# Windowed attention and a gated feed-forward layer on one core: pooled scores in one product, shorter turns, another order of the outputs

## The reference

```python
# q, k, v: (4 batches, 8 heads, 576 positions, 64)
q_d, k_d, v_d = (x.reshape(B, H, 144, 4, D).mean(axis=3) for x in (q, k, v))
out_up = np.repeat(softmax(q_d @ k_d.T / 8) @ v_d, 4, axis=2)        # pooled attention
scores = np.where(abs(i - j) < 4, q @ k.T / 8, -1e9)                 # a band of 7 keys
x = out_up + softmax(scores) @ v                                     # local attention
x = x.transpose(0, 2, 1, 3).reshape(2304, 512)
h = x @ w_in                                                         # 512 -> 2048
out = (h * tanh(softplus(h))) @ w_out                                # 2048 -> 512
```

## Time and profile before

| | |
|---|---|
| three timed runs | 502.68, 503.96, 504.90 us; median 503.96 |
| the profiled execution | 502.42 us, span from first to last instruction 500.6 us |
| PE busy | 486.8 us (97%) |
| weight loads busy | 431.9 us (86%) |
| DVE, ACT, POOL busy | 231.2, 204.3, 118.7 us |
| mean granted clock of TensorE | 0.996 of full |
| DMA | 39.61 MB, mean 79 GB/s |

### The profile page before, as it was taken

The page is one execution under the profiler, slowest core; times in us unless marked ns, Lnnn a source line. Parts: engine busy times, 40 slices in busy tenths (PEclk is TensorE's granted clock), DMA queues, the critical chain, the costliest instruction groups (busy, mean ns, idle before and its releaser), DMA issues.

```text
span 500.6 us, 10568 instructions
## 1 busy us (share of the span) xinstructions
PE 486.8 (97%) x4260; PEld 431.9 (86%) x4260; DVE 231.2 (46%) x469; ACT 204.3 (41%) x434; POOL 118.7 (24%) x188
## 2 busy tenths in 40 slices
PE   7789999999999999999999999999999999999997
PEld 6578888988988988889889889898998898999996
DVE  4755878454553534434625435345155253222221
ACT  3778366654623424625424534244254241211111
POOL 5899614223303203033032022021020210000000
PEclk9989999999999999999999999999999999999999
DMA  8993083132330230530301301101121000100001
GB/s 262 295 368 109 1 310 110 47 92 96 98 106 13 95 106 0 169 104 3 106 8 49 118 1 54 58 1 56 43 77 56 6 17 2 54 10 1 0 1 63
DMA packets 22704, 39.61 MB, mean 79 GB/s; under 512 B 2688, under 2 KB 8576, under 8 KB 22656
## 3 DMA queue, kind: packets, MB, share of 16 engines
q1 hardware_dynamic: 22656, 38.94, 24.3%
HBM read 34.21 MB, written 4.72 MB: 78 GB/s over the span
## 4 chain that ended last, share of the span: by engine, by line
PE 89%; DMA 4%; SPq 2%; POOL 2%; ACT 1%; issue 1%; DVE 0%; ACTq 0%; POOLq 0%
PE banks L685 39%; PE banks L700 39%; PE banks L645 3%; PE banks L632 2%; PE banks L570 2%; PE banks L603 2%; DMA w_out_raw<-in_w_out 2%; PE banks L614 1%; DMA v_in<-in_v 1%; PE banks L585 1%; SPq L318 1%; DMA k_t<-in_k 1%; SPq L330 1%; POOL v_half L450 1%; POOL v_pool L450 0%
## 5 line engine op out<-in xcount | busy, mean ns | idle before, releaser
L920 DVE CAST g_high<-banks 128x384 fp32r<-128x384 f32 x96 | 53.3, 556 | 172.7 <-PE banks L700 128.5
L685 PE MATMUL banks<-x_high,w_in_high 128*128 128x384 f32 x384 | 130.6, 340 | 2.0 <-DVE g_low L922 2.0
L685 PE MATMUL banks<-x_high,w_in_low 128*128 128x384 f32 x384 | 129.4, 337 | 0.0
L685 PE MATMUL banks<-x_low,w_in_high 128*128 128x384 f32 x384 | 128.9, 336 | 0.0
L1114 ACT ACTIVATE banks<-banks 128x384 f32<-128x384 f32 x96 | 45.4, 476 | 202.3 <-PE banks L685 202.1
L700 PE MATMUL banks<-w_out_high,g_high 128*128 128x512 f32 x288 | 115.2, 400 | 0.0
L700 PE MATMUL banks<-w_out_high,g_low 128*128 128x512 f32 x288 | 113.5, 394 | 0.0
L700 PE MATMUL banks<-w_out_low,g_high 128*128 128x512 f32 x288 | 113.1, 393 | 0.0
L459 POOL TENSOR_TENSOR prob<-prob,small 128x432 f32<-128x432 f32 x24 | 22.6, 941 | 260.3 <-DVE small L884 260.3
L685 PEld LDWEIGHTS banks<-x_high,w_in_high 128*128 128x128 f32 x384 | 72.2, 188 | 6.1 <-DVE g_low L922 2.8
L685 PEld LDWEIGHTS banks<-x_low,w_in_high 128*128 128x128 f32 x384 | 72.1, 188 | 2.9
(11 more groups left out here) (70 smaller groups left out, 470.9 us busy)
## 6 DMA issues: line engine op xcount, KB each, us to landing
v_win<-in_v_win SPq DMA_DIRECT2D x24, 256.0 KB, 2.9
v_in<-in_v SPq DMA_DIRECT2D x32, 160.0 KB, 4.0
k_t<-in_k SPq DMA_DIRECT2D x16, 290.0 KB, 3.6
q_t<-in_q SPq DMA_DIRECT2D x24, 192.0 KB, 3.3
out<-stage SPq DMA_DIRECT2D x17, 256.0 KB, 2.3
k_win<-in_k_win SPq DMA_DIRECT2D x20, 216.0 KB, 3.4
w_out_raw<-in_w_out SPq DMA_DIRECT2D x16, 256.0 KB, 5.9
w_in_raw<-in_w_in SPq DMA_DIRECT2D x16, 256.0 KB, 9.6
```

Source lines behind the costliest of these rows:

```text
L685: last = nc.tensor.matmul(hidden[:, g % HB, 0:TB], w, x[:, k, cols], start=(k == 0 and i == 0), stop=(k == KT - 1 and i == 2))
L920: nc.vector.tensor_copy(g_high[:, g % GB], x).then_inc(g_rounded, 1)
```

## The change

Three edits on PE and one on ACT. `pooled_scores` gives both tiles to one product as 128 weight columns where they share a batch, and goes tile by tile as before where they don't. `turn_band` streams 112 columns of the identity in place of 128 and reads 112 rows. `turn_pooled` uses a plain product in place of a transposing one, with the identity's columns 0 to 47 and 64 to 111 streamed, so that the empty columns are left out and the four results lie side by side, 96 columns each; `copy_pooled` then reads 384 adjacent columns. In `outputs` the loop over the keys' half (array rows) is inside the loop over the heads (array columns).

```diff
 # pooled_scores
-                    for t in range(GT):
-                        half, place_of = pooled_of(n, t)
+                    one = batch(n, 0) == batch(n, 1)
+                    for tiles in (slice(0, GT),) if one else (slice(0, 1), slice(1, GT)):
+                        half, place_of = pooled_of(n, tiles.start)
                         for h in range(2):
                             rows = slice(D * h, D * (h + 1))
-                            last = nc.tensor.matmul(b[WK * t:WK * (t + 1), h], s["q_pool"][rows, t],
+                            last = nc.tensor.matmul(b[WK * tiles.start:WK * tiles.stop, h],
+                                                    s["q_pool"][rows, tiles].rearrange("p t q -> p (t q)"),
                                                     k_pool[rows, half, place_of], start=True, stop=True)
 # turn_band
-                        last = nc.tensor.transpose(b[:, 0, P * i:P * (i + 1)],
-                                                   s["prob"][:, 2 * i:2 * i + 2].rearrange("p w k -> p (w k)"), ident)
+                        last = nc.tensor.transpose(b[:, 0, P * i:P * i + GR],
+                                                   s["prob"][0:GR, 2 * i:2 * i + 2].rearrange("p w k -> p (w k)"),
+                                                   ident[0:GR, 0:GR])
 # turn_pooled
-                            at = P * (2 * h + kh)
-                            last = nc.tensor.transpose(b[0:GH, 1, at:at + GR],
-                                                       s["prob_pool"][:, h, kh * GH:(kh + 1) * GH],
-                                                       ident[0:GR, 0:GR])
+                            at = GU * (2 * h + kh)
+                            last = nc.tensor.matmul(b[0:GH, 1, at:at + GU],
+                                                    s["prob_pool"][:, h, kh * GH:(kh + 1) * GH],
+                                                    ident[0:GR, 0:P].rearrange("p (t q) -> p t q", q=WK)[:, 0:GT, 0:GQ],
+                                                    start=True, stop=True)
 # outputs
-                            for r in range(2):
-                                keys = slice(WK * r, WK * r + KW)
-                                for h in range(2):
+                            for h in range(2):
+                                for r in range(2):
+                                    keys = slice(WK * r, WK * r + KW)
 # copy_pooled
-                    nc.scalar.copy(s["prob_pool_t"][:].rearrange("g h k t q -> g (h k) t q"), turned(b[0:GH, 1])
+                    nc.scalar.copy(s["prob_pool_t"][:].rearrange("g h k t q -> g (h k t q)"), b[0:GH, 1, 0:4 * GU]
```

## The result

The changed kernel takes 511.16 us as a median of four runs (510.53 to 513.49), the kernel before 504.28 in the same comparison, so the medians lie 6.9 us apart. The ratio, as estimated from the runs, is 1.0145, with a 95% interval from 1.0107 to 1.0182; that is 7.3 us more (5.4 to 9.2). The forecast was 511.3, or 7.3 more. The profiled execution took 511.73, its span is 509.9, 9.3 more than that of before.

The account below looks back on a forecast made before the run. PE, busy for 97% of the span, bounds the kernel. Pooled turns +5.4, band turns -0.95, scores +2.5, order 0 and start +0.35 give +7.3 us: 509.8 profiled, 511.3 as a median, range 508 to 514.5.

Parts of the forecast that it names:

- Pooled turns: PE's pooled turns: eight plain records replace four transposing products, +0.285 us a unit, 5.4 us over 19 units.
- Rival A: Pooled turns: a plain product takes one record of 84 ns, total +0.7 us, median 504.7, not slower; 4%.
- Band turns: PE's band turns: 112 columns in place of 128, -0.05 us a unit, -0.95 us over 19 units.
- Pooled scores: One product for both tiles: new change of tile size and open weight load, +0.21 us, 2.5 us over 12 units.
- the open load: Pooled scores: loading 128 weight columns unhidden, as at L700, 0.11 us of the 0.21.
- B: Pooled scores: 64x128 tiles need no drain and their weights load unseen, total +4.7 us, 508.7; 12%.
- C: Pooled scores: the two row tiles run one after the other, 3 us more, 514.3; 6%.
- Order of the outputs: Windows' outputs: array rows alternating first changes nothing, since four tiles already run at once; 0 us.
- What lies ahead of waits: Places where PE's time is not the path: the 0.7 us wait hides unit 5's +0.235; unit 4's turns pass on.
- The start's 0.35: Start of the kernel: unit 0's pooled scores and unit 3's turns delay it by +0.35 us, of -0.1 to +0.9.
- unit 4's 0.24 us: Unit 4's turns: their added time, +0.235 us, lies ahead of SP's issues at 61.93 and passes on.
- A half clock behind 35 us: Sign of being wrong: a new stretch at half clock behind 35 us would cost time that no step has.

Follow-up runs that it names:

- e1: Kernel before with only the pooled turns as plain products of 96 columns and the adjacent copy on ACT; median 509.68 us, ratio 1.0125.
- e5: Kernel before with the pooled turns as plain products of 112 columns at their old places; 510.08 us, one run.
- e2: Kernel before with only the pooled scores in one product for both tiles where they share a batch; median 506.87 us, ratio 1.0073.
- e9: Kernel before, burst reordered: pooled outputs of the previous unit, then pooled scores, band scores, windows' outputs; median 501.21 us, ratio 0.9980.
- e4: Kernel before with only the order of the outputs changed, array rows alternating first; median 504.48 us, ratio 1.0015.
- e12: The kernel before, unchanged, run again for a second trace; 502.17 us, one run.
- e3: Kernel before with only the band turns cut to 112 columns and rows; median 504.53 us, ratio 1.0016.
- e7: Kernel before with the previous unit's pooled outputs moved ahead of the band scores; median 512.41 us, ratio 1.0149.

## Why the prediction was right

**Pooled turns**, 19 units of 0.285 us: the step held. The trace has 0.29 us a unit (9.69 against 5.08 us in the stretch), e1 shows the edit alone, e5 that two records and their columns are the reason. The step from the last turn to L700 is the same for both forms within 5 ns, so it falls out of the difference. Rival A, one record a product, is out: 192 records. e1's 83 ns are the 84 that were worked out from another shape.

**Band turns**, -0.05 us a unit: held, -0.81 us in the 16 units of the stretch.

**Pooled scores**, 12 units of 0.21 us: the mechanism held, the size was a little high. Gap and longer product are 0.11 and 0.08 us, 2.26 us for the 12. The part of the term that was too high is the open load, which was taken from L700 at 0.11 us: in the trace's nanoseconds the distance from the group's first start to the first start of its second round grew from 133 to 227, by 0.09 us, and the group has four records less to start, which gives back 0.01. Rivals B (no drain) and C (the row tiles one after the other) are out: there is a gap, and the four records start in two pairs. The Trainium skill's rule that a change of tiling mode drains the engine (TensorEngine Tiling (Array Packing), Key Properties) agrees with these runs: e2 adds such a change and has a gap of 0.11 us where there was none, e9 takes one away and its bursts are 0.12 us shorter.

**Order of the outputs**, 0: held (e4). The Trainium skill's rule that a load overlaps only where the row group differs (TensorE: Matmul & The Clock Gate, Part 3, "What overlaps and what doesn't") would have let the new order gain; the 0.61 us of e4 do not agree.

**What lies ahead of waits.** Here the working was incomplete. It counted the first of the two waits of the earlier trace rows as a place where time can be lost unseen, and then set nothing against it. It stood at 73.21 us in the kernel before:

```profile
73.21 0.44 PE L685 MATMUL banks<-x_high,w_in_high 128*128 128x384 f32 x1 [0.80 <-DVE g_low L922]
```

The start's 0.35 and unit 4's 0.24 us lie ahead of it. Had it taken them up, the forecast would have been 6.7 us more and not 7.3; the measured interval holds both. Whether it would have is open. The changed kernel has no wait left between 45 and 440 us, and its 4.2 us of delay at unit 4's turns are 3.1 at unit 6's band scores (82.32 against 79.20), so some of the delay was taken up. But the unchanged kernel, too, has neither of the two waits in its second trace (e12), only one of 0.5 us: they belong to one execution. The loads of w_out in the chain of the earlier trace rows differ as well. The last of them landed 14.3 us behind the start of unit 4's windows' outputs in the first trace of the kernel before, 12.2 in e12 and 11.9 in the changed kernel.

**What no step had.** A half clock behind 35 us was named as a thing that would cost time without being foreseen. It came in the profiled run, where it moves unit 7's turns by most of their 3.39 us. The 9.3 us between the spans against 6.9 between the medians have another reason: the profiled execution of the kernel before, at 502.42 us, was 1.9 below its median of 504.28, that of the changed kernel 0.6 above its own. And L704's groups give back 0.34 us in the stretch (L700's in e3 0.41), cause open.

**How much of the hit is luck.** The mechanisms are shown by the stretch, but that the median came out 0.14 us from the forecast is luck. In the stretch the forecast's own terms make 16 x 0.285 - 16 x 0.05 + 12 x 0.21 = 6.3 us, and 5.69 were measured: 0.3 less by the pooled scores and 0.3 by L704's groups. What the medians have above that lies in the first 105 us and in the scatter of four runs each, either of which can move more than the 0.6 us that were missing.

## What to carry to other kernels

Fewer columns need not be a gain where the form of the product changes: a plain f32 product left two records in these traces, a transposing one a single record at the same price per column, and that turned 14% fewer columns into 90% more time (0.32 to 0.61 us). On an array that is split into tiles, count the changes of tile size in the stream and not only the products: merging products two by two into wider ones cost 0.19 us a burst, and reordering so that equal tiles stand together gained 0.12, but only once other products stood between the engine's results and the products that wait for them. Where whole runs scatter by more than an edit is worth, measure a stretch of the trace in which the bound engine never waits.

## What the hardware showed beyond that

- Products on four 64x64 tiles ran together in either order of rows and columns, each four products in a row going to the four tiles: 0.61 us for 32 records in both (e4).
- In a stretch where PE does not wait, two executions of one program agree to 10 ns in 306.62 us (e12). The scatter of this kernel's runs, from 500.7 to 510.5 us over 75 runs, follows the granted clock; that it arises in the first 105 us is inferred from the traces, since the 75 runs have none.
- An engine's wait on its own results has a price: from the last start of the pooled scores it took 0.46 us until the waiting outputs began (e7), where without a wait, and with a change of tile size, it takes 0.21 (L585 to L632).
